# Half-size weight pieces in four buffers, ScalarE making the first dense x, and twelve unread products behind the scatters

## The reference

```python
# 1: linear attention with decay
for t in range(S):
    cur = einsum('bhd,bhe->bhde', u * kt, vt)
    y[:, :, t] = einsum('bhd,bhde->bhe', rt, state + cur)
    state = w * state + einsum('bhd,bhe->bhde', kt, vt)
# 2: top-1 mixture of 8 experts, D = 384, F = 1024
e = argmax(x @ w_gate);  gate = softmax(x @ w_gate)[e]
out[token] = gate * (relu(x @ w1[e]) @ w2[e])
# 3: dense layer, d_ff = 2048
h = x @ w_in;  return maximum(0.01 * h, h) @ w_out
```

## Time and profile before

| | us |
|---|---|
| median of 3 runs | 836.39 |
| lowest, highest | 830.72, 836.74 |
| the profiled execution | 825.21 |
| its span, first to last instruction | 823.5 |

### The profile page before, as it was taken

One profiled execution on the slowest core, in us unless ns is written; L12 is line 12 of the kernel. 1 busy time (PEld: TensorE's weight loads), 2 busy tenths in 40 slices (PEclk: granted clock), 3 DMA queues, 4 the chain that ended last, 5 costly groups with the idle time before them and its releaser, 6 DMA issues.

```text
span 823.5 us, 17748 instructions
## 1 busy us (share of the span) xinstructions
PE 771.5 (94%) x7200; PEld 707.7 (86%) x7200; DVE 335.7 (41%) x658; ACT 215.1 (26%) x436; POOL 335.3 (41%) x338
## 2 busy tenths in 40 slices
PE   9889889469998989999899999999999999999995
PEld 8778777459998989999889889989988998998994
DVE  7868755613233133223544333433433433433332
ACT  2224433311122112111122232222232223232221
POOL 6568855637767677976991010010010001001001
PEclk9999989779999999999999999999999999999998
DMA  4757654354665355356430000010000000001000
GB/s 145 225 159 208 182 164 148 117 125 136 109 124 150 91 146 157 103 146 146 115 117 1 1 38 1 1 39 1 1 38 0 0 0 38 0 0 39 1 1 39
DMA packets 42611, 66.91 MB, mean 81 GB/s; under 512 B 11413, under 2 KB 31797, under 8 KB 42549
## 3 DMA queue, kind: packets, MB, share of 16 engines
q1 hardware_dynamic: 28944, 50.76, 22.6%
q10 hardware_dynamic: 10533, 5.80, 3.7%
q0 software_dynamic: 3072, 9.45, 3.1%
HBM read 51.42 MB, written 14.59 MB: 80 GB/s over the span
## 4 chain that ended last, share of the span: by engine, by line
PE 79%; POOL 9%; issue 5%; DMA 3%; DVE 2%; ACT 0%; ACTq 0%; POOLq 0%; SPq 0%; DVEq 0%
PE bank L1174 24%; PE bank L1153 24%; PE bank L1114 7%; PE bank L1098 7%; POOL w_lo L134 5%; PE ps_y L833 3%; POOL w_hi L130 2%; DMA stage<-in_moe_w 2%; PE ps_y L818 2%; PE ps_x L790 2%; PE ps_s L770 2%; PE ps_x L786 2%; PE ps_l L854 1%; PE ps_x L845 1%; PE ps_m L804 1%
## 5 line engine op out<-in xcount | busy, mean ns | idle before, releaser
L1042 POOL DMA_INDIRECT out_rows<-rows,ids_i x24 | 23.1, 962 | 358.7 <-ACT rows L1253 353.2
L1318 DVE TENSOR_TENSOR h_lo<-gf,h_hi 128x512 fp32r<-128x512 f32 x96 | 70.2, 732 | 227.4 <-ACT h_hi L1244 227.4
L134 POOL TENSOR_TENSOR w_lo<-stage,w_hi 128x768 fp32r<-128x768 f32 (+1 forms) x70 | 146.4, 2092 | 5.8
L1174 PE MATMUL bank<-w_hi,h_hi 128*128 128x384 f32 x384 | 130.4, 339 | 0.0
L1174 PE MATMUL bank<-w_lo,h_hi 128*128 128x384 f32 x384 | 129.3, 337 | 0.0
L1174 PE MATMUL bank<-w_hi,h_lo 128*128 128x384 f32 x384 | 129.1, 336 | 0.0
L1240 ACT ACTIVATE hc<-bank 128x512 f32<-128x512 f32 x96 | 57.4, 597 | 273.1 <-PE bank L1153 273.1
L1153 PE MATMUL bank<-x_hi,w_hi 128*128 128x512 f32 x288 | 114.0, 396 | 2.3 <-DVE x_lo L1300 2.3
L1153 PE MATMUL bank<-x_lo,w_hi 128*128 128x512 f32 x288 | 114.3, 397 | 0.0
L1153 PE MATMUL bank<-x_hi,w_lo 128*128 128x512 f32 x288 | 113.9, 395 | 0.0
L1281 DVE SCALAR_TENSOR_TENSOR h_lo<-bank,h_hi 128x416 fp32r<-128x416 f32 x64 | 37.7, 591 | 149.5 <-ACT h_hi L1220 149.5
(11 more groups left out here) (170 smaller groups left out, 1185.5 us busy)
## 6 DMA issues: line engine op xcount, KB each, us to landing
stage<-in_moe_w SPq DMA_DIRECT2D x24, 512.0 KB, 6.0
stage<-in_moe_w SPq DMA_DIRECT2D x32, 384.0 KB, 3.1
rows<-x_rows ACTq DMA_DIRECT2D x9, 625.6 KB
x_rows<-pad_row SPq DMA_DIRECT2D x32, 156.4 KB
k_u<-in_k SPq DMA_DIRECT2D x48, 96.0 KB, 3.0
r_u<-in_r SPq DMA_DIRECT2D x48, 96.0 KB, 2.7
v_u<-in_v SPq DMA_DIRECT2D x24, 192.0 KB, 3.5
stage<-in_moe_w_in SPq DMA_DIRECT2D x6, 512.0 KB, 4.3
```

Of the source, the lines that this page charges most:

```text
L134: i = eng.tensor_tensor(w_lo[:, buf, off:off + cols], stage[:, h, 0:cols], w_hi[:, buf, off:off + cols].bitcast(F32), ALU.subtract)
L1174: i = pe.matmul(ps_o[t][:, 0:D], x[:, f % NB, t * P:(t + 1) * P], ww[:, 1, o:o + D], start=f == 0 and x is h_hi and ww is w_hi, stop=f == ...
L1318: dve.tensor_tensor(h_lo[:, f % NB, :], gf[:, f % 2, :], h_hi[:, f % NB, :].bitcast(F32), ALU.subtract).then_inc(gl_ok, 1)
```

## The change

Three parts, in words, and then the core of the diff.

1. `PIECE` is 512 and `stage` has `NS` = 4 buffers, so it is as large as before. An expert has 14 pieces, 6 of 512 columns and 8 of 384; `w_in` has 12 and `w_out` 16. Piece `n` may be loaded when piece `n - 4` has been split. The units of stage 1 that loaded or split one piece now do two. The loads move the same bytes. The count of the loads, of the splits and of the ticks doubles. The w1 and w_in loads have rows of 2 KB where they had 4 KB; the w2 and w_out rows stay at 1.5 KB.
2. For the first dense group ScalarE makes the three chunks of `x_hi`, after its part of the last expert group; VectorE makes only `x_lo`.
3. Ahead of the first expert group TensorE waits for `scattered` and then makes 12 products of `ident` by `ident` that nobody reads.

```diff
-    PIECE = 1024
+    PIECE = 512
+    NS = 4
@@ expert_pieces
-        p = [(c * FE, FE, w1e[:, c * P:(c + 1) * P, :].rearrange("o p f -> p o f")) for c in range(DC)]
-        p += [(DC * FE + f * D, 2 * D, w2e[:, f * P:(f + 2) * P, :].rearrange("o (f p) d -> p (o f) d", p=P))
-              for f in range(0, FC, 2)]
+        p = [(c * FE + h * PIECE, PIECE, w1e[:, c * P:(c + 1) * P, h * PIECE:(h + 1) * PIECE].rearrange("o p f -> p o f"))
+             for c in range(DC) for h in range(FE // PIECE)]
+        p += [(DC * FE + f * D, D, w2e[:, f * P:(f + 1) * P, :].rearrange("o p d -> p o d")) for f in range(FC)]
@@
-        stage = sb("stage", [P, 2, PIECE])
+        stage = sb("stage", [P, NS, PIECE])
@@ load_piece
-            if not isinstance(n, int) or n >= 2:
-                eng.wait_ge(split_done, n - 1)
+            if not isinstance(n, int) or n >= NS:
+                eng.wait_ge(split_done, n - (NS - 1))
@@ attention
-            LOAD_AT = {4: 2, 5: 3, 8: 4, 9: 5, 12: 6}
-            SPLIT_AT = {4: 0, 5: 1, 8: 2, 9: 3, 12: 4, 13: 5, 16: 6}
+            LOAD_AT = {4: (4, 5), 5: (6, 7), 8: (8, 9), 9: (10, 11), 12: (12, 13)}
+            SPLIT_AT = {4: (0, 1), 5: (2, 3), 8: (4, 5), 9: (6, 7), 12: (8, 9), 13: (10, 11), 16: (12, 13)}
@@ layers, on_tensor
                 pe.wait_ge(grouped, 1)
                 pairs, last = pairs_of(pe), last_of(pe)
+                pe.wait_ge(scattered, SCATTERS * C)
+                for _ in range(12):
+                    pe.matmul(ps_h[0][:, 0:P], ident[:, :], ident[:, :], start=True, stop=True)
                 group(0, 0)
@@ layer2
-                        pe.wait_ge(split_done, w_out_at + (f // 2 + 1))
+                        pe.wait_ge(split_done, w_out_at + (f + 1))
@@ on_scalar
+                last = last_of(act)
+                act.wait_ge(y_copied, last * DC)
+                for d in range(DC):
+                    at = (NG - 1) * (G * P) + U
+                    act.activation(x_hi[:, 0, d, :], z_t[:, d, at:at + G * P], ACT.Copy).then_inc(xh_ok, 1)
@@ on_vector, x_split
-                        dve.tensor_scalar(x_hi[:, b, d, :], z, 1.0, None, ALU.mult).then_inc(xh_ok, 1)
+                        if not isinstance(g, int) or g > 0:
+                            dve.tensor_scalar(x_hi[:, b, d, :], z, 1.0, None, ALU.mult).then_inc(xh_ok, 1)
```

More of the change, by code:

```diff
@@ L62, in w_out_pieces @@
     def w_out_pieces():
-        return [(f * D, 2 * D, moe2_w_out[f * P:(f + 2) * P, :].rearrange("(f p) d -> p f d", p=P))
-                for f in range(0, FFC, 2)]
+        return [(f * D, D, moe2_w_out[f * P:(f + 1) * P, :].unsqueeze(1)) for f in range(FFC)]
     NPE = len(expert_pieces(0))
-    ENDS = (DC - 1, NPE - 1)
+    NP1 = DC * FE // PIECE
+    ENDS = (NP1 - 1, NPE - 1)
     NPI = len(w_in_pieces())
     NPO = len(w_out_pieces())
+    assert NPE * 2 % NS == 0 and NPI % NS == 0
     ctx = ExitStack()
@@ L93, in build_program @@
         tick = sb("tick", [P, 4])
-        staged = [sem(f"staged{i}") for i in range(2)]
+        staged = [sem(f"staged{i}") for i in range(NS)]
         split_done = sem("split_done")
@@ L124, in split_piece @@
             off, cols, _ = piece
-            nh = n // 2 if isinstance(n, int) else None
+            nh = n // NS if isinstance(n, int) else None
             eng.wait_ge(staged[h], 16 * (nh + 1) if nh is not None else h_count(n, h))
@@ L142, in h_count @@
         def h_count(n, h):
-            return (n - h) * 8 + 16
+            return (n - h) * (16 // NS) + 16
         def attention():
@@ L352, in on_sync @@
                 pc = expert_pieces(0)
-                for n in range(2):
+                for n in range(NS):
                     issue_piece(sp, n, n, pc[n])
@@ L362, in on_sync @@
                         zero_rows(n)
-                    if g in LOAD_AT:
-                        n = LOAD_AT[g]
-                        issue_piece(sp, n, n % 2, pc[n])
+                    for n in LOAD_AT.get(g, ()):
+                        issue_piece(sp, n, n % NS, pc[n])
             def on_gpsimd(pool):
@@ L463, in on_gpsimd @@
                             scatter(c - 2, b)
-                    if g in SPLIT_AT:
-                        n = SPLIT_AT[g]
-                        split_piece(pool, n, n % 2, 0, pc[n], n in ENDS)
+                    for n in SPLIT_AT.get(g, ()):
+                        split_piece(pool, n, n % NS, 0, pc[n], n in ENDS)
                 for c in (C - 2, C - 1):
@@ L1003, in weights @@
                     for i, piece in enumerate(expert_pieces(e)):
-                        issue_piece(sp, n * NPE + i, (b * NPE + i) % 2, piece)
+                        issue_piece(sp, n * NPE + i, (b * NPE + i) % NS, piece)
                 sp.wait_ge(grouped, 1)
@@ L1016, in on_sync @@
                 for n, piece in enumerate(w_in_pieces()):
-                    issue_piece(sp, base + n, n % 2, piece)
+                    issue_piece(sp, base + n, n % NS, piece)
                 base = base + NPI
                 for n, piece in enumerate(w_out_pieces()):
-                    issue_piece(sp, base + n, n % 2, piece)
+                    issue_piece(sp, base + n, n % NS, piece)
                 sp.wait_ge(stored, STORES * NG)
@@ L1026, in weights @@
                     for i, piece in enumerate(expert_pieces(0)):
-                        if not isinstance(n, int) and i in (0, DC):
+                        if not isinstance(n, int) and i in (0, NP1):
                             pool.wait_ge(l2_mm if i else h_mm, n * FC - FC)
                             carry_wait(pool, 2)
-                        split_piece(pool, n * NPE + i, (b * NPE + i) % 2, b, piece, i in ENDS)
+                        split_piece(pool, n * NPE + i, (b * NPE + i) % NS, b, piece, i in ENDS)
                 def scatter(g):
@@ L1053, in on_gpsimd @@
                 for n, piece in enumerate(w_in_pieces()):
-                    if n in (0, DC):
+                    if n in (0, NP1):
                         pool.wait_ge(l2_mm if n else h_mm, last * FC)
                         carry_wait(pool, 2)
-                    split_piece(pool, base + n, n % 2, 0, piece, n in (DC - 1, NPI - 1))
+                    split_piece(pool, base + n, n % NS, 0, piece, n in (NP1 - 1, NPI - 1))
                 base = base + NPI
@@ L1067, in on_gpsimd @@
                         carry_wait(pool, 2)
-                    split_piece(pool, base + n, n % 2, 1, piece, False)
+                    split_piece(pool, base + n, n % NS, 1, piece, False)
                 pool.wait_ge(ids_ok, 1)
```

## The result

| | before | after |
|---|---|---|
| median, us (20 runs each) | 833.97 | 836.09 |
| lowest, highest | 825.94, 849.97 | 830.06, 846.91 |
| the profiled execution | 825.21 | 840.86 |

The account below looks back on a forecast made before the run. TensorE, 94% busy, was taken as the bound, with weights late until group 4. Terms 4.5 + 1.85 + 2.3 + 1.9 + 1.0 = 11.5 us off the 836.4 median gave 824.9, stated as 825.0; range 815 to 836.

Parts of the forecast that it names:

- The sum: Whole kernel: weight waits 4.5, low clock after 1.85, x_lo wait 2.3, low clock after 1.9, group 0 1.0: 11.5 us gained.
- stage 1 ends later than 171.8: Sign set beforehand: if stage 1 ends later than 171.8 us in the profile, the prediction is wrong.
- more than the sum: Rival: timed runs' extra 11 us over the profiled one are longer load waits, partly taken by deeper buffers: 817; chance 0.08.
- the weight stream: Expert stage: expert 1 split by 201 us, then 28.9 us an expert on GpSimd, under the 29.2 limit; both w2 waits go.
- GpSimd becomes the bound: Rival, expert stage: 30.6 us an expert, expert 7 done 8.1 us late, gain only 3.4 us, 833.0; chance 0.20.
- The slow rival: Expert stage: half a load takes as long as a whole one while `move_ids` runs; 32.5 us an expert, 844.4; chance 0.08.
- The dense start: First dense group: ScalarE's copies remove the 2.3 us x_lo wait and 1.9 us of low clock; `w_out` leads by one us.
- The unread products: Ahead of group 0: twelve products, 3.7 to 7.3 us long, let it start at a higher clock; 1.0 us gained.
- Stage 1: Before the expert groups: seven more pieces cost GpSimd 3.5 us, put at 0 on the path, 3.5 as the bound.

Follow-up runs that it names:

- the second profile: Kernel before, no edit, timed against itself and profiled again: ratio 1.002. Of the changed kernel: the same kernel timed and profiled again, ratio 1.0092.
- part 2 alone: Only ScalarE making x_hi of the first dense group, put on the kernel before: ratio 0.9949.
- part 3 alone: Only the twelve unread products, put on the kernel before: ratio 1.0025.
- the four profiles with half pieces: Half-size pieces in four buffers alone on the kernel before (1.0067), the change (1.0063), the change without unread products (1.0067), the change again (1.0092).
- the last measurement: The changed kernel timed again against the kernel before, beside three other kernels on one chip: ratio 1.0092.
- the two later pairs: Kernels without and with the unread products, against the kernel before: three large buffers with ScalarE's x_hi 0.9871 and 0.9892; the change 1.0067 and 1.0092.
- three buffers: Kernel before with ScalarE's x_hi and, from expert 1, three buffers of up to 1152 columns, six pieces an expert: ratio 0.9952, later 0.9871.

## Why the prediction was wrong

**What was there to gain.** The sum took 4.5 + 1.85 us of weight waits and of low clock behind them from one execution, and its expert stage was indeed 6.5 us longer than the 228.0 us of the second profile, which has none of these waits. The other two profiles with the same loads and splits lie between: 231.7 us in part 2's, with one wait of 2.2, and 230.4 in part 3's, with one of 2.5. So some 3 us were there to gain on average. The gap of 11 us between that execution and the median was in sight, and one rival read it as longer load waits. It was stage 1 at the low clock: 14.7 us longer in the second profile, so that "stage 1 ends later than 171.8" could say nothing about the change. The rival "more than the sum" rested on that reading and falls.

**The step that failed is the weight stream: a start at 201 us and then 28.9 us an expert.** Of the 28.9, splitting at 26.2 us was right (pieces of 2.10 and 1.72 us). The load waits were not. I let one load an expert be held up by `move_ids`, for 8.15 us, and the others land in 3.1; that left 1.9 us. The 8.15 was only the part of a landing on the chain; in that same profile landings of weight loads took up to 10.0 us (least, median and most, for those issued from 150 to 420 us):

```profile
DMA to landing us min/median/max: 2.8/3.5/10.0
```

And in the profile after, five 256 KB loads are in flight with each `move_ids` and land after 6.7 us in the median, beyond the 5.1 to 6.3 us by which they are issued ahead. Why a 1.6 KB DMA does this was not tried, and no kernel with half pieces was run without it. Two things followed. Expert 1 was to be split 201 - 171.8 = 29.2 us after group 0's transposes began; it was done after 32.4 us, with 4.1 us of load waits instead of 1.9. That alone moves the pace up to which TensorE would not wait from 29.2 to 28.7 us an expert. And the load waits were 2.4 us an expert in the profile of record and 3.1 in the second, and the pace 29.6, 30.0, 30.6 and 30.9 us in the four profiles with half pieces, all above either limit. In the four with whole pieces and the loads of before it was 28.3 us in the mean. So the saving in load waits was about 2.6 us an expert (from 5.3 to 2.7, two profiles each), the price in splitting 3.5, and the stream became slower by 2 us an expert, of which 1 us is in neither term.

**From this to the 5 us.** The expert stage was 233.6, 236.1, 241.3 and 243.1 us with half pieces, against 234.5, 228.0, 231.7 and 230.4 with whole ones: 7 us more in the mean, with a wide spread. Part 2 gives 4 us back. That leaves 3 us in the profiles, where the timed runs have 5 in the result and 8 in the last measurement; profiles and timed runs are different executions.

This is the rival "GpSimd becomes the bound", which had 0.20. At 30.6 us an expert it still had 3.4 us gained, as it took the stream to start at 201 and all of the 11.5 us to be there; 5 us were lost.

**The slow rival** had the right direction and half of the mechanism. Half a load does take about as long as a whole one while `move_ids` runs (5.7 us against 6.0 in the median). But it put the price on the count of the loads, and doubling that costs nothing (0.9987), while doubling the splits costs 21 us; its 32.5 us an expert was not reached.

By the Trainium skill, "DMA: Bandwidth & Descriptors", section Anatomy of one DMA, each DMA has a fixed cost; the section gives its figures for DMAs issued by GpSimd, and the loads here are issued by SyncE. By its formula, as an estimate, 192 KB take 2.5 us and 256 KB 2.6; the profile after has 2.4 for 192 KB, and 2.9 for 256 KB without a `move_ids`. Serial loads would have added 14 us an expert. In no run here did that show, as the loads overlap: an estimate from the medians in the profile after is 6 x 5.7 + 8 x 2.4 = 53 us of landing in 29.6 us an expert.

**The dense start.** For part 2 alone 4.2 us were forecast, and 4.2 measured, with an interval from 1 to 7; the profile has 4.6, and no wait for `x_lo`. The mechanism was right; that the size fits so well is partly luck. In the changed kernel the lead of one us of `w_out` was not there, since the stream was late: the wait of 2.0 us at L1180 took the place of that for `x_lo`, in the profile of record. In the second profile the dense stage is 413.6 and the gain is there.

**The unread products.** 1.0 us forecast in group 0. Group 0 took 26.8, 26.8, 27.5 and 27.5 us in the four profiles with them and 27.8 to 28.7 in the others: 1.0 us less for part 3 alone, 0.3 and 0.5 in the two later pairs. The 24 instructions took 5.5 us, between the 3.7 and 7.3 forecast, and ended before the rows landed. None of it can be seen in time.

**Stage 1.** Put at 0, and 186.3 against 186.5 us is in line with that, though stage 1 varies by more than the 3.5 us in question.

## What to carry to other kernels

Splitting pieces in two buys depth and pays the fixed cost of every operation twice. Before doing it, put the sum of the engine that works on the pieces beside the pace it has to keep; with 26.2 of 28.0 us there is hardly room left for a wait. If depth is what is wanted, add a buffer of the same size where memory has become free, and make the pieces fewer: here that took every weight wait out of the trace, though whether it gives time beyond part 2's gain was not settled. Look which other DMAs are in flight beside the loads, too; a small one can be what makes them late. And before a wait is booked as a gain, look whether a second execution of the same kernel has it.

## What the hardware showed that was not expected

TensorE's clock falls in stage 1 while it is busy. The window from 80 to 90 us in the first profile of before and in part 2's, whose stage 1 is the same code (columns as in the earlier trace rows):

```profile
80.00:90.00 10.00, 7.90 (x254) 6.58 (x246) 6.62 (x17) 3.34 (x9) 9.10 (x10) 1.00 0.82 237
```

```profile
80.00:90.00 10.00, 8.63 (x151) 7.14 (x151) 4.10 (x11) 1.52 (x4) 5.77 (x7) 0.52 0.52 162
```

The same stretch runs mostly at 1.2 GHz in one execution and at 2.4 in another, with TensorE 79 and 86% busy. In the profile after, TensorE was 100% busy from 140 to 150 us at a clock of 0.58. What tips it was not tried; it is the largest thing open in this kernel, some 14 us between two runs of the same code.

And a DMA of 416 numbers of 4 bytes, 1.6 KB, raised the median landing of 512 KB loads from 3.6 to 6.0 us. It goes with the loads that are in flight beside it: w1's in before, w2's with three buffers.
